# Weight sums in pieces on GpSimd, and a new order at the seam of two layers, at the last loads and at the last sums

## The reference

```python
x = attention(q, k, v, bias)                  # (2304, 512)
h = np.maximum(np.maximum(x @ w1, x @ w2), x @ w3)      # d_ff 768
x = h @ w_out                                 # first layer's output, (2304, 512)
h = x @ w_in                                  # d_ff 2048
g = np.where(h >= 1, h, np.where(h <= -1, 0.0, (h + 1) ** 2 / 4.0))
out = g @ w_out2                              # (2304, 512)
```

## Time and profile before

| | us |
|---|---|
| median of 3 runs | 1020.13 (1017.62 to 1020.18) |
| profiled execution | 1020.09 |
| its span, first to last instruction | 1018.3 |
| TensorE busy (matmuls) | 991.1, 97% |
| VectorE, ScalarE, GpSimd busy | 616.4, 509.4, 347.4 |
| mean granted TensorE clock | 0.989 |

### The profile page before, as it was taken

How to read it: one execution, slowest core, us unless ns; L and a number is a source line. 1 busy time by engine, 2 the same in 40 slices (tenths; PEclk the granted TensorE clock), 3 DMA queues, 4 the chain that set the end, 5 groups by cost and what they waited for, 6 DMA issues and landing times.

```text
span 1018.3 us, 23175 instructions
## 1 busy us (share of the span) xinstructions
PE 991.1 (97%) x8832; PEld 897.6 (88%) x8832; DVE 616.4 (61%) x1509; ACT 509.4 (50%) x1034; POOL 347.4 (34%) x522
## 2 busy tenths in 40 slices
PE   6979999999999999999999998999999999999998
PEld 3567777777767999999999998999999999999998
DVE  8957667666683242324231315677777877778776
ACT  8968778788793321212121213444554554545443
POOL 1059888888874878677300000000000000000000
PEclk9979999999999999999999999999999999999999
DMA  5982534425312464665510067866657667666772
GB/s 130 268 240 55 161 72 119 109 53 154 95 34 75 133 223 170 230 235 209 222 84 0 9 223 309 271 215 205 212 190 220 199 215 210 204 211 188 226 219 72
DMA packets 122149, 169.71 MB, mean 167 GB/s; under 512 B 67008, under 2 KB 84416, under 8 KB 120256
## 3 DMA queue, kind: packets, MB, share of 16 engines
q1 hardware_dynamic: 121952, 168.37, 53.0%
q10 hardware_dynamic: 96, 0.00, 0.0%
HBM read 129.64 MB, written 38.70 MB: 165 GB/s over the span
## 4 chain that ended last, share of the span: by engine, by line
PE 72%; DVE 2%; ACT 1%; issue 0%; DVEq 0%; ACTq 0%
PE ps L1265 22%; PE ps L1333 20%; PE ps L1359 18%; PE ps L1292 7%; PE ps L1216 2%; PE ps L1156 2%; PE ps L1177 1%; PE ps L1191 0%; DVE x_lo L979 0%; DVE tb L1095 0%; PE ps L1130 0%; ACT tb L866 0%; ACT ta L862 0%; DVE s_sb L926 0%; DVE g_lo L1107 0%
## 5 line engine op out<-in xcount | busy, mean ns | idle before, releaser
L1265 PE MATMUL ps<-x_hi,w_all 128*128 128x384 f32 x864 | 227.2, 336 | 3.0 <-DVE x_lo L979 1.8
L1333 PE MATMUL ps<-x_hi,w_all 128*128 128x256 f32 x1152 | 219.3, 283 | 1.2 <-DMA w_all<-win_scratch 1.2
L1359 PE MATMUL ps<-w_all,g_hi 128*128 128x256 f32 x1008 | 185.9, 284 | 2.6 <-ACT ta L862 2.4
L1333 PEld LDWEIGHTS ps<-x_hi,w_all 128*128 128x128 f32 x1152 | 184.8, 192 | 1.6 <-DMA w_all<-win_scratch 1.6
L1333 PE MATMUL ps<-x_lo,w_all 128*128 128x256 f32 x576 | 163.0, 283 | 0.0
L1265 PEld LDWEIGHTS ps<-x_hi,w_all 128*128 128x128 f32 x864 | 157.5, 189 | 5.3 <-DVE x_lo L979 2.3
L1359 PEld LDWEIGHTS ps<-w_all,g_hi 128*128 128x128 f32 x1008 | 158.3, 193 | 3.0 <-issue 2.6
L926 DVE CUSTOM_DVE_ANT_0 s_sb<-ps,bias_h 128x576 f32<-128x576 f32 (+1 forms) x160 | 114.8, 754 | 71.5 <-PE ps L1156 53.7
L1265 PE MATMUL ps<-x_lo,w_all 128*128 128x384 f32 x432 | 145.1, 336 | 0.0
L1359 PE MATMUL ps<-w_all,g_lo 128*128 128x256 f32 x504 | 143.1, 284 | 0.0
L586 POOL TENSOR_SCALAR probs<-probs,row_inv 128x576 f32<-128x576 f32 (+1 forms) x160 | 120.8, 766 | 18.7 <-DVE row_inv L956 18.1
(11 more groups left out here) (115 smaller groups left out, 1806.5 us busy)
## 6 DMA issues: line engine op xcount, KB each, us to landing
w_all<-win_scratch SPq DMA_DIRECT2D x144, 512.0 KB, 4.3
wt_scratch<-w_all SPq DMA_DIRECT2D x8, 1792.0 KB, 6.8
w_all<-wt_scratch SPq DMA_DIRECT2D x6, 1792.0 KB, 7.5
bias_scratch<-p_t SPq DMA_DIRECT2D x36, 296.0 KB, 4.6
win_scratch<-w_all SPq DMA_DIRECT2D x8, 1024.0 KB, 7.0
raw<-in_moe_w_out SPq DMA_DIRECT2D x22, 256.0 KB, 7.1
bias_h<-bias_scratch SPq DMA_DIRECT2D x16, 288.0 KB, 4.2
raw<-in_moe_w SPq DMA_DIRECT2D x18, 256.0 KB, 3.0
```

The costliest lines, as they stand in the source:

```text
L1265: last = pe.matmul(ps[:, bank, 0:BLK], w[:, at:at + P], x[:, kt, :], start=(kt == 0 and n == 0), stop=(kt == KT - 1 and n == 2))
L1333: last = pe.matmul(ps[:, n_bank(n), f * SBT:(f + 1) * SBT], w_all[:, at + lo:at + lo + P], x[:, s, :], start=(kt == 0 and i == 0), stop=(k ...
L1359: last = pe.matmul(ps[:, bank, 0:HD], x[:, n % 2, g * P:(g + 1) * P], w_all[:, at + lo:at + lo + HD], start=(j == 0 and m == 0), stop=(j = ...
```

## The change

It has five parts.

1. GpSimd's `split_in` copies in two instructions of 512 columns and subtracts in four of 256; `split_out` copies and subtracts in seven instructions each, of 256 columns.
2. At the seam, TensorE makes `d_products(0)` before the first layer's last `c_y`. For this `high_xd` and `low_xd` of the first block stand inside the last item of the first layer, ahead of `gc_hi` on ScalarE and ahead of `gc_lo` on VectorE, and the last `y_copy` stands inside step 0 of the second layer.
3. `n_bank` gives banks 3, 2 and 0 to steps 0, 1 and 2 and on. The wait for `d_cp` 3 ahead of `d_sums(0)` is replaced by one for `d_cp` 2 ahead of the product in bank 2, the last of the seven.
4. `load_wt(5)` comes in quarters too, and the quarters of 5, 6, 7 follow window loads 8 to 11, 12 to 15, 16 to 19. SP's wait for the last `c_item` stays where it was.
5. In the last block of output VectorE reads products 5, 3 and 4 from PSUM, the two ScalarE copies go, and the last 256 KB store becomes two of 128 KB, the first of them after `d_post` 5.

```diff
-            return n if n < 3 else 0
+            return (3, 2)[n] if n < 2 else 0
...
-        PIECES = {6: {5: 0, 7: 1, 9: 2, 11: 3}, 7: {13: 0, 14: 1, 15: 2, 16: 3}}
+        PIECES = {j: {m: m % 4 for m in range(4 * j - 12, 4 * j - 8)} for j in (5, 6, 7)}
...
-            for j in range(1, NPAIR - 2):
+            for j in range(1, 5):
                 sp.wait_ge(c_item, c_freed(j))
                 load_wt(j, 0, 1)
             sp.wait_ge(c_item, c_freed(NF1))
...
+                    if t == 0 and b == NSB - 1:
+                        sp.wait_ge(d_post, 7 * b + 5)
+                        sp.dma_start(out[at:at + P, HD:DM], o_sb[:, 0, HD:DM]).then_inc(d_out, 16)
+                        sp.wait_ge(d_post, 7 * b + 7)
+                        sp.dma_start(out[at:at + P, 0:HD], o_sb[:, 0, 0:HD]).then_inc(d_out, 16)
+                    else:
+                        sp.wait_ge(d_post, 7 * b + done)
+                        sp.dma_start(out[at:at + P, :], o_sb[:, t, :]).then_inc(d_out, 16)
...
-                for j in (6, 7):
+                for j in PIECES:
...
-                pool.tensor_scalar(win_st[:, :, 0:half], x, 1.0, 1.0, ALU.mult, ALU.mult).then_inc(win_hi, 1)
+                for f in range(2):
+                    last = pool.tensor_scalar(win_st[:, f, 0:half], x[:, f, :], 1.0, 1.0, ALU.mult, ALU.mult)
+                last.then_inc(win_hi, 1)
                 pool.wait_ge(win_hi, j + 1)
-                pool.tensor_tensor(win_st[:, :, half:2 * half], x, win_st[:, :, 0:half].bitcast(F32),
-                                   ALU.subtract).then_inc(w_ok, 1)
+                for f in range(2):
+                    for c in range(0, half, PIECE):
+                        last = pool.tensor_tensor(win_st[:, f, half + c:half + c + PIECE], x[:, f, c:c + PIECE],
+                                                  win_st[:, f, c:c + PIECE].bitcast(F32), ALU.subtract)
+                last.then_inc(w_ok, 1)
...
-                parts = ((B11, 4, raw[:, 1, :]), (T1, 3, acc_sb[:, :]))
-                for i, n, x in parts:
-                    last = pool.tensor_scalar(wt_st[:, i * HD:(i + n) * HD], x, 1.0, 1.0, ALU.mult, ALU.mult)
+                parts = ((B11, b11), (T2, t2), (B21, b21), (B22, b22), (T1, t1), (T3, t3), (T4, t4))
+                for i, x in parts:
+                    last = pool.tensor_scalar(wt_st[:, i * HD:(i + 1) * HD], x, 1.0, 1.0, ALU.mult, ALU.mult)
...
ScalarE, in c_block, after its copy of bank 0:
+                    if last and ft == NF1 - 1:
+                        act.wait_ge(c_h, 3 * NF1 * NBLK)
+                        for kt in range(KT):
+                            high_xd(0, kt)
                     act.wait_ge(c_m2, n + 1)
...
ScalarE, in step n of the second layer, after its square (L866):
+                if n == 0:
+                    y_copy(NBLK)
+                    act.wait_ge(c_y_ok, KT * NBLK)
                 act.wait_ge(d_g, n + 1)
...
-            sums_rest(NSB - 1)
...
VectorE, in c_block, after the second maximum (L1021):
+                    if last and ft == NF1 - 1:
+                        for kt in range(KT):
+                            low_xd(0, kt)
                     dve.wait_ge(c_g_hi, n + 1)
...
VectorE, sums_rest:
+                if b == NSB - 1:
+                    p5, p3, p4 = (ps[:, bank, 0:HD] for bank in (P5_BANK, P3_BANK, P3_BANK + 1))
+                    dve.wait_ge(d_acc, 6 * b + 5)
+                else:
+                    dve.wait_ge(d_acc_cp, 3 * b + 2)
...
+                if b == NSB - 1:
+                    dve.wait_ge(d_acc, 6 * b + 6)
+                else:
+                    dve.wait_ge(d_acc_cp, 3 * b + 3)
                 dve.wait_ge(d_post, 7 * b + 4)
                 dve.tensor_tensor(o_12, p3, o_12, ALU.add).then_inc(d_post, 1)
+                if b == NSB - 1:
+                    dve.wait_ge(d_item, NPAIR * NSB)
...
VectorE, in step n of the second layer, after s4 (L1102):
+                if n == 0:
+                    y_copy(NBLK)
+                    dve.wait_ge(c_y_ok, KT * NBLK)
...
TensorE:
             blocks(pe, c_block)
-            c_y(NF1 * NBLK - 1, NF1 - 1, False, True)
...
-                if n == 0:
-                    pe.wait_ge(d_cp, 3)
                 for i, (bank, g, w) in enumerate(PRODUCTS):
+                    if n == 0 and bank == n_bank(1):
+                        pe.wait_ge(d_cp, 2)
...
             for n in range(ND):
                 d_products(n)
+                if n == 0:
+                    c_y(NF1 * NBLK - 1, NF1 - 1, False, True)
```

More of the change, by code:

```diff
@@ L514, in store_out @@
                 for t, done in ((1, 6), (0, 7)):
-                    sp.wait_ge(d_post, 7 * b + done)
                     at = b * SBT + t * P
-                    sp.dma_start(out[at:at + P, :], o_sb[:, t, :]).then_inc(d_out, 16)
+                    if t == 0 and b == NSB - 1:
[6 more added lines that the diff above has]
+                        sp.dma_start(out[at:at + P, :], o_sb[:, t, :]).then_inc(d_out, 16)
             for m in range(WRING, NF2 * NSB):
                 load_win(m)
-                for j in (6, 7):
+                for j in PIECES:
                     if m in PIECES[j]:
@@ L526, in _ @@
             store_out(NSB - 1)
-            sp.wait_ge(d_out, 32 * NSB)
+            sp.wait_ge(d_out, 32 * NSB + 16)
         @block.gpsimd
@@ L646, in split_out @@
                     pool.wait_ge(wt_out, 16 * j)
-                parts = ((B11, 4, raw[:, 1, :]), (T1, 3, acc_sb[:, :]))
-                for i, n, x in parts:
-                    last = pool.tensor_scalar(wt_st[:, i * HD:(i + n) * HD], x, 1.0, 1.0, ALU.mult, ALU.mult)
+                parts = ((B11, b11), (T2, t2), (B21, b21), (B22, b22), (T1, t1), (T3, t3), (T4, t4))
+                for i, x in parts:
+                    last = pool.tensor_scalar(wt_st[:, i * HD:(i + 1) * HD], x, 1.0, 1.0, ALU.mult, ALU.mult)
                 last.then_inc(wt_hi, 1)
                 pool.wait_ge(wt_hi, j + 1)
-                for i, n, x in parts:
-                    last = pool.tensor_tensor(wt_st[:, TCOLS + i * HD:TCOLS + (i + n) * HD], x,
-                                              wt_st[:, i * HD:(i + n) * HD].bitcast(F32), ALU.subtract)
+                for i, x in parts:
+                    last = pool.tensor_tensor(wt_st[:, TCOLS + i * HD:TCOLS + (i + 1) * HD], x,
+                                              wt_st[:, i * HD:(i + 1) * HD].bitcast(F32), ALU.subtract)
                 last.then_inc(w_ok, 1)
@@ L794, in _, with high_xd @@
             act.wait_ge(o_ok, PAIRS)
+            def high_xd(b, kt):
+                if b and kt >= XRING - KT:
+                    act.wait_ge(d_x_used, (KT - 2) * (b - 1) + kt - 1)
+                act.activation(xd_hi[:, x_slot(b, kt), :], xT[:, kt, x_cols(b)], ACT.Copy).then_inc(d_x_hi, 1)
             def c_block(b, first, last):
@@ L823, in _ @@
             blocks(act, c_block)
[L824 to L836, removed]
             act.wait_ge(w_ok, U1 + U2)
@@ L1007, in _, with low_xd @@
             output(GROUPS - 1, 1)
+            def low_xd(b, kt):
+                dve.wait_ge(d_x_hi, KT * b + kt + 1)
+                dve.tensor_tensor(xd_lo[:, x_slot(b, kt), :], xT[:, kt, x_cols(b)],
+                                  xd_hi[:, x_slot(b, kt), :].bitcast(F32), ALU.subtract).then_inc(d_x_ok, 1)
             def c_block(b, first, last):
@@ L1035, in _ @@
             blocks(dve, c_block)
[L1036 to L1047, removed]
             dve.wait_ge(w_ok, U1 + U2)
+            dve.wait_ge(c_g_ok, NF1 * NBLK)
             o_11, o_12 = o_sb[:, 1, 0:HD], o_sb[:, 1, HD:2 * HD]
```

2 lines of the change are left out of this document (removed).

## The result

The changed kernel takes 1012.82 us (median of 4 runs, 1012.16 to 1014.19), the kernel before beside it 1019.85 (4 runs, 1017.62 to 1020.18). The ratio is 0.9938, with a 95% interval of 0.992 to 0.9956: 7.0 us less where 8.7 were forecast. A second set of six runs gave 1012.95 beside 1019.08 for before (0.9943, 0.9924 to 0.9962). The profiled execution took 1012.26 us, span 1010.2, mean clock 0.996, against 1020.09, 1018.3 and 0.989: 7.8 us less.

What follows compares the result with a forecast made beforehand. TensorE, busy 97% of the span, was taken as the bound, so only its waits and half clock could be won: 3.86 + 4.6 + 0.2 = 8.7 us off 1020.1 gives 1011.4 us, range 1009.3 to 1015.5.

Steps and rivals of the forecast that it cites:

- First layer: Narrower GpSimd instructions end VectorE's `x_lo` delay near 463 us: gain 3.86 us, bounds 0 and 3.9.
- Seam: Between first and second layer, new order, banks and loads remove waits and half clock: gain 4.6 us, bounds 2.0 to 5.7.
- the one stall at window load 4: At the seam, the load issued behind output product 35 lands late: new stall 1.0 us, bounds 0.8 to 2.2.
- End: After the last matmul, PSUM reads and a halved last store gain 0.2 us, bounds -0.3 and 0.6.
- Steady part: Second layer's window loads and weight quarters fit the DMA engines: cost zero, bounds 0 and 1 us.
- GpSimd's later end: GpSimd ends 10 to 19 us later, covered by over 90 us before its loads are needed: cost nothing.
- the likeliest case: Whole kernel: the forecast itself, chance 0.63, with a time of 1010.2 to 1012.5 us.
- The margin of half a microsecond: First layer near 464 us: the fourth `x_lo` tile ends at 464.3, TensorE takes it at 464.8.
- A: Seam: load 4 lands late, a 2.2 us stall and half clock follow; gain there 2.0, total 1014.0 us; chance 0.18.
- B: First layer: four `x_lo` tiles beside pieces take over 4.3 us, the 3.86 us loss stays, total 1015.3; chance 0.12.
- C: Second layer: window loads and quarters outrun the DMA engines, 9 us of stalls, 1022 us or more; chance 0.03.
- D: Seam: `d_g_ok` 1 or `d_cp` 3 some 3 us late, and `x_lo` tiles late too; about 1018.5 us; chance 0.04.

Runs made afterwards that it cites:

- pieces_late: Changed kernel with fourteen fills delaying GpSimd by about 11 us; no timed median, first layer 282.92 us, four `x_lo` tiles 4.08 us.
- wide_late: Kernel before with ten fills ahead of GpSimd's first sums, its instructions still wide; no timed median, first-layer loss 7.4 us.
- banks_quarters: Kernel before with banks 3, 2, 0, the changed wait, and sums' weights 5 to 7 in quarters; no timed median, seam 17.01 us.
- seam_quarters: Changed kernel without GpSimd's pieces and without its last sums; 1013.97 us against 1018.52 for before, ratio 0.996.
- tail_alone: Kernel before with only the last output block's PSUM reads and halved last store; no timed median, end 4.33 us for 4.52.
- pieces_alone: Kernel before with only GpSimd's split instructions in pieces; 1017.28 us against 1017.65 for before, ratio 0.9992.
- quarters_alone: Kernel before with only the loads of sums' weights 5 to 7 changed to later quarters; no timed median, seam 20.75 us.
- seam_alone: Kernel before with only the new seam order, banks 3, 2, 0 and changed wait, weights 5 in one load; 1018.40 us, ratio 1.0003.
- banks_alone: Kernel before with only banks 3, 2, 0 for steps 0 to 2 and the changed wait; no timed median, seam 17.37 us.
- load4_first: Changed kernel with SP's wait for the last `c_item` moved behind window loads 4 and 5; 1011.59 us, ratio 0.9936 to before.

## Why the prediction was right, and where it was off

**The mechanism held in all three places.** First layer: 3.86 us forecast, 3.86 found, all of it from part 1, by GpSimd's width. (That the two figures are equal is no second measurement: both are what the one trace of before had above the floor. What was confirmed is that all of it goes.) Seam: 4.6 forecast, 4.66 found, with the one stall at window load 4 that was forecast (1.0 us; 0.83 found, landing 3.6 us as for a load alone) and no other. End: 0.2 forecast, 0.17 found. Steady part: 0 forecast, +0.01 found. GpSimd's later end is hidden. No tile of `x_lo` took more than 1.09 us (1.2 was the mark), and all items of the first layer take 8.32 us. The time, 1012.82 us, lies inside the range of 1009.3 to 1015.5 and just above the 1010.2 to 1012.5 of the likeliest case. One bound was too tight: four tiles beside 256-column instructions were to take at most 3.75 us, and took 3.83 in the changed kernel and 4.08 in `pieces_late`. The margin of half a microsecond covered it, barely in the second case.

**What was mis-sized is the term for the first layer, and less so the seam's, because I took them from one execution that had paid both in full.** Every kernel with wide GpSimd instructions stalls at block 3 for 1.2 to 1.8 us. What differs more is the granted clock behind the stall. In four of seven executions (`wide_late` not counted) it stayed at full and the loss was 1.5 to 2.1 us; in three (before, `banks_quarters`, `seam_quarters`) it fell, and the loss was 3.6 to 3.9. No edit in these seven touches anything ahead of the last block of the first layer, so at block 3 they are seven executions of one program: the difference lies between executions, not kernels. An example of each kind: in `tail_alone` the stall is 1.80 us and the window of 4 us behind it is at full clock:

```profile
468.09 0.44 PE L1279 MATMUL ps<-x_hi,w_all 128*128 128x384 f32 x1 [1.80 <-DVE x_lo L984]
```

```profile
470.00:474.00 4.00, 4.00 (x25) 1.00 1.02 394
```

In before and in `seam_quarters` the stall is 1.83 and 1.76 us, and the clock falls; in the latter it is 0.70 over 4 us:

```profile
466.39 0.44 PE L1265 MATMUL ps<-x_hi,w_all 128*128 128x384 f32 x1 [1.83 <-DVE x_lo L979]
...
466.78 0.45 PE L1266 MATMUL ps<-x_hi,w_all 128*128 128x384 f32 x1 [1.76 <-DVE x_lo L979]
```

```profile
466.00:470.00 4.00, 3.22 (x12) 0.70 0.93 291
```

The mean loss over the seven is 2.6 us. The seam in the old order is alike: 21.04, 21.16 and 20.75 where the clock fell behind the wait (before, `pieces_alone`, `quarters_alone`: 0.59 and 0.63 over 4 us in the last two), 19.69 and 19.67 where it did not (`tail_alone`, `wide_late`). Their mean, 20.5, is 4.1 above the changed kernel's. So a typical gain is 2.6 + 4.1 + 0.2 = 6.9 us, and the medians say 7.0 and 6.1. The weights come from five to seven executions, so this is an estimate. The step that was off is the prediction's "I take the whole 3.86 as gained" and its "I forecast from it": what one execution happened to pay was taken as what every execution pays. That the profiled execution stood on the median of three runs was no comfort: in 40 further runs, in three sets, before had medians of 1017.65, 1018.52 and 1019.08.

**Open.** `pieces_alone` gained 0.4 us by the medians (-0.8 to 2.4), less than the 2.6 of the traces. Its ten runs had a mean granted clock of 0.9930, the nineteen of before beside them 0.9941: the estimate from that is 1.1 us more lost to the clock with the pieces than without, and no trace says at which place. The other sets put part 1 higher: 0.9943 and 0.9938 for the whole change against 0.996 for `seam_quarters`, which lacks parts 1 and 5, are 1.7 and 2.2 us for these two parts, an estimate across sets with intervals of about as much. The untouched attention alone spreads by 4 us, and I have one trace of each kernel's runs (two of the changed one); what part 1 typically saves isn't settled.

**The rivals.** A (the load behind the output product, 0.18) did not come in the changed kernel; it is what the new order does without quarters, at a higher price than A had (`seam_alone`). B (late all the same, 0.12) fell with `pieces_late`. C (loads outrun the engines, 0.03) fell: 373 GB/s were moved from 632 to 635 without a wait. D fell: the third copy and the low parts came as added up, with no wait for either.

## What to carry to other kernels

Where one execution shows a stall with half clock behind it, split the term: the stall is paid every time, the clock only sometimes, and a forecast for a median takes the second by its share of executions. Change a bank or a wait before an order: five lines gave 3.7 of the seam's 4.7 us, and the reordering gave nothing until the transfer ahead of its load was cut up. Where VectorE's two-input instructions wait for GpSimd's, as here, the width of one instruction is the longest wait of the other; to see whether width or phase saved a block, shift the phase on purpose.

## What the runs showed of the hardware that I had not expected

- The length of a stall does not tell whether the clock falls behind it. After TensorE stood 1.76 to 1.85 us at block 3 it was full in two executions (`tail_alone`, `wide_late`) and fell in three (before, `banks_quarters`, `seam_quarters`); behind 1.83 us at block 2 of `wide_late` it fell too. At the seam it fell behind waits of 2.15, 2.40, 3.54 and 3.67 us (`pieces_alone`, before, `seam_alone`, `quarters_alone`) and stayed full behind 2.52 and 3.15 (`tail_alone`, `wide_late`). After 1.17 and 1.60 us (`seam_alone`, `quarters_alone`, `banks_alone`) it stayed full, and so it did after waits of 0.7 to 1.3 us at the seam. The fall cost 1.5 to 1.8 us at block 3 (3.63 to 3.86 us of loss, against the 2.08 of `tail_alone` after a like stall) and 1.1 to 1.5 at the seam in the old order.
- A 512 KB window load landed after 3.4 to 3.7 us with nothing issued in the 5 us ahead of it (load 4 in eight executions), and after 4.8 to 5.0 us in four executions, and once each 5.5 and 6.3, with 1792 KB issued 3.6 to 5 us ahead.
- The attention part, with the same instructions everywhere, took 326.4 to 330.4 us. The granted clock from 60 to 80 us differs between executions (0.58 in `quarters_alone`, the longest, and 0.75 in `load4_first`, the shortest), but it doesn't order them: with 0.83 there the changed kernel took 328.6. The cause isn't settled. The spread is as large as each of the two gains of this change, so a total of one execution can't stand for any of them.
